# Sparse attention, MLP and routed experts on one core: denominators behind the first strikes, early outputs copied a step later, the next expert split two tiles ahead, ScalarE preparing the first tile's mask in every step

## The chip, the core and the metric

One core of one Trainium2 chip. The metric is the device time of one launch in microseconds; the median of several runs counts. TensorE multiplies matrices, VectorE (DVE in the rows), ScalarE (ACT) and GpSimd (POOL) work element by element, SyncE (SP) issues transfers. "Granted clock" is TensorE's clock as a share of its full 2.4 GHz; its other level is 1.2 GHz.

## What is computed

```python
# attention: q, k, v are 4 x 8 x 576 x 64
scores = scale * np.matmul(q, k.transpose(0, 1, 3, 2))
kth = np.partition(scores, -32, axis=-1)[..., -32:-31]
mask = scores >= kth
attn = exp(where(mask, scores, -1e9) - max);  attn /= attn.sum(-1)
x = (attn @ v), rows of 8 heads x 64 = 512, 2304 tokens
# MLP, 512 -> 2048 -> 512
h = x @ w_in;  g = maximum(h, 0) + log1p(exp(-abs(h)));  x = g @ w_out
# experts: 8, one per token by argmax of x @ w_gate, 512 -> 1024 -> 512
out[mask] = gate_w[mask] * (maximum(x[mask] @ w1[e], 0) @ w2[e])
```

Everything is float32. Large products are made of three: each operand is split into a rounded high part and the rest, its low part, and high x high, high x low and low x high are added.

## The kernel before

The scores are worked off in 72 blocks of 2 tiles (128 query rows x 576 keys each). A block passes the engines as a pipeline over steps i, written out by hand for each engine. In step i TensorE makes the scores of block i+1, transposes the probabilities of block i-2 (`turn_probs`, L536) and multiplies them with v (`times_v`, L554). ScalarE copies scores out (`scores_out`, L808), takes exponentials of block i-1 (`exponentials`, L823), multiplies block i-2 by its reciprocal denominators (`normalise`, L829), copies transposed probabilities (`probs_out`, `prT`, L836) and the output x (`x_out`, L843). VectorE finds the 32 largest scores of each row of block i: four rounds of the 8 largest (`maxima`, L1077), with those found struck out between rounds (`strike`, L1083). It also sums the exponentials and takes reciprocals (`reciprocals`, L1094 and L1097) and makes the low part of x (`x_low`, L1089). Its instructions run in the order in which they are written; so do those of every engine.

The mask that puts all but the 32 largest far below is made in one of two ways. GpSimd alone: compare and multiply (L1422, into `pr`), then add the scores (L1425). Or ScalarE first makes a large value for what lies below the limit (`cut_off`, L816) and GpSimd subtracts it (L1418). `cuts(n)` says which tiles of block n have the second way: both for n below 8, then tile 0 of even blocks, none of odd blocks. `tiles_of(n)` puts tile 1 first where only tile 0 is cut.

From step MLP_AT = 10 on the MLP runs in the same steps: group g of 256 tokens takes eight steps u = 0 to 7, one unit of the hidden layer each (`up`, `down`, on TensorE; `h_hi` on ScalarE L868, softplus and `h_lo` on GpSimd L1430 and L1436). `up(g, 0)` waits for the low part of the last block of its tokens (semaphore `x_split`). Steps 1 and 2 of the next group transpose two finished token tiles and compute their gate logits (`TURNS`); at step 0 of the next group ScalarE copies the group's result (`x2tok`, L889). Before step 10 ScalarE and GpSimd split the MLP's weights (L874, L880).

After the blocks come the routed experts. Tokens are sorted into tiles of 128 of one expert each; tile T has `rank_i[T]`, the place of its expert in the order. Tiles are gathered, multiplied (`e_up`, `e_down`, L669 to L671, with transposes of the hidden layer between, L699) and scattered by GpSimd (`scatter`: the indices are copied, L1517, then an indirect transfer is issued, L1520). Weights of the next expert are loaded into a second buffer; ScalarE casts their high part (`w_hi`, L912), VectorE makes the low part (`wbuf`, L1122). `next_expert(eng, T, split)` reads two ranks and does `split` if tile T+1 belongs to a later expert. In tile T ScalarE does `e_relu_out` (L947), `xs_out(T+1)`, the split of w1 and w2, `e_h_out` (`hrT_hi`, L953); VectorE does the low half of w1, `h_low` (L1271), the low half of w2, `relu(T+1)` (L1260), `xs_low(T+2)`, `y_out` (L1281). Here 19 tiles are in use, with two experts.

Of the kernel before, what the change touches and what calls it, by code (L numbers as in the profile page):

```python
# [20 lines left out]
def build(nc, q, k, v, w_in, w_out, w_gate, w1, w2, out):  # L21
# [68 lines left out]
    FREE = MLP_AT - 2  # L90

    def cuts(n):
        return (0, 1) if n < FREE else ((0,) if n % 2 == 0 else ())

    def cuts_before(n):
        return sum(len(cuts(x)) for x in range(n))
# [20 lines left out]
    with ExitStack() as ctx:  # L117
        def sb(name, shape, dt=F32):
            return ctx.enter_context(nc.sbuf_tensor(name, shape, dt))

        def sem(name):
            return ctx.enter_context(nc.semaphore(name))
# [121 lines left out]
        first_tile = sb("first_tile", [P, E])  # L244
        rank_e = sb("rank_e", [P, NTAB])
        rank_i = sb("rank_i", [P, COLS], I32)
        src_i = sb("src_i", [P, COLS], I32)
        dstf = sb("dstf", [P, NTAB])
        wrap = sb("wrap", [P, NTAB])
# [36 lines left out]
        lanes_ready, slots_raw, tables_ready = sem("lanes_ready"), sem("slots_raw"), sem("tables_ready")  # L286
        star_ready, tiles_ready, ranks_ready = sem("star_ready"), sem("tiles_ready"), sem("ranks_ready")
        onehot_ready = sem("onehot_ready")
        shift_ready = sem("shift_ready")
        xs_turned, xs_copied = sem("xs_turned"), sem("xs_copied")  # L290
        e_h_raw, e_relu, e_h_turned = sem("e_h_raw"), sem("e_relu"), sem("e_h_turned")
# [5 lines left out]
        def is_block(n):  # L297
            return 0 <= n < BLOCKS
# [34 lines left out]
        def next_expert(eng, T, split):  # L333

            rank, rank_next = (eng.value_load(rank_i[0:1, bass.ds(T + x, 1)], min_val=0,
                                              max_val=E - 1) for x in range(2))
            with eng.If(rank_next > rank):
                split(rank_next)

        def live_below(eng):  # L340
            tiles = eng.value_load(tend_i[0:1, E - 1:E], min_val=MOST, max_val=NTILE)
# [155 lines left out]
        def _(pe):  # L497
# [60 lines left out]

            def up(g, u, amid=()):
                n = UNITS * g + u  # L560
                if u == 0:
                    pe.wait_ge(x_split, PAIRS * 2 * (g + 1))
                if g == 0:
                    pe.wait_ge(wi_split, u + 1)
                if n:
                    pe.wait_ge(h_copied, n)
                if turns:
                    pe.wait_ge(logits_copied, turns)
                ps = psum[:, 5, 0:2 * WIDE].rearrange("p (a c) -> p a c", a=2)
                for part in range(2):  # L570
                    f = slice(part * P, (part + 1) * P)
                    for kk in range(KD):
                        if (part, kk) in amid:
                            amid[part, kk]()
                        first, last = kk == 0, kk == KD - 1
                        hi, lo = x_parts[:, g % 2, 0, kk, :], x_parts[:, g % 2, 1, kk, :]
                        nc.tensor.matmul(ps[:, part, :], wi_hi[:, u, kk, f], hi, start=first, stop=False)  # L577
                        nc.tensor.matmul(ps[:, part, :], wi_hi[:, u, kk, f], lo, start=False, stop=False)  # L578
                        mm = nc.tensor.matmul(ps[:, part, :], wi_lo[:, u, kk, f], hi,  # L579
                                              start=False, stop=last)  # L580
                mm.then_inc(h_raw, 1)
# [199 lines left out]
            turn_xs(1, 1)  # L781
            turn_h(0)
            e_up(1, rank_first)
            e_down(0, 0, rank_first, {KE // 2: slots_late, KE // 2 + 1: lambda: turn_h(1)}, halves=True)
            e_down(1, 1, rank_first, {KE - 2: lambda: turn_xs(2, 2)})
            pe.wait_ge(tiles_ready, 1)
            e_up(2)
# [15 lines left out]
        def _(act):  # L803
# [114 lines left out]
            def split_w2(rank):  # L918
                split_half(rank, w2_loaded, KD * EF, WLEN, w2_hi)

            def split(rank):
                split_w1(rank)
                split_w2(rank)

            def first_w1(n, half):
                at, rows = slice(n * 512, (n + 1) * 512), slice(half * KD // 2, (half + 1) * KD // 2)
                act.wait_ge(w1_loaded[0] if n else w1_first, 32)
# [31 lines left out]
            for i in range(-AHEAD, TAIL):  # L959
                now, late = is_block(i - 1), is_block(i - 2)  # L960
                if i < MLP_AT:
                    if late:
                        normalise(i - 2, 0)
                        normalise(i - 2, 1)
                    if now:
                        for t in cuts(i - 1):
                            cut_off(i - 1, t)
                    scores_out(i + AHEAD, 0)
                    scores_out(i + AHEAD, 1)
                    if late:  # L970
                        probs_out(i - 2, 0)
                    if wo_unit(i) is not None:
                        split_wo(wo_unit(i))
                    if now:
                        exponentials(i - 1, 0)
                    if late:
                        probs_out(i - 2, 1)
                    if now:
                        exponentials(i - 1, 1)
                    if wi_unit(i) is not None:  # L980
                        split_wi(wi_unit(i))
                    if late:
                        x_out(i - 2)
                    continue
                if up_at(i - 1):
                    h_high(*up_at(i - 1))
                if is_block(i + AHEAD):
                    scores_out(i + AHEAD, 0)
                    scores_out(i + AHEAD, 1)
                if late:  # L990
                    normalise(i - 2, 0)
                    normalise(i - 2, 1)
                if now:
                    for t in cuts(i - 1):
                        cut_off(i - 1, t)
                if up_at(i):
                    rectify(*up_at(i))
                if late:
                    probs_out(i - 2, 0)
                if now:  # L1000
                    exponentials(i - 1, 0)
                if late:
                    probs_out(i - 2, 1)
                if i in TURNS:
                    turn_out(TURNS[i][1], 5)
                if up_at(i):
                    logarithm(*up_at(i))
                if now:
                    exponentials(i - 1, 1)
                if down_at(i) and down_at(i)[1] == UNITS - 1:  # L1010
                    down_out(down_at(i)[0])
                if late:
                    x_out(i - 2)
                if i in TURNS:
                    logits_out(TURNS[i][1], 5)
# [37 lines left out]
            e_relu_out(1)  # L1053
            e_h_out(1)
            xs_out(2)
            act.wait_ge(tiles_ready, 1)
            next_expert(act, 1, split)
            _, live = live_below(act)

            def tile(T, place, live):  # L1060
                e_relu_out(T)
                with live(T + 1):
                    xs_out(T + 1)
                    next_expert(act, T, split)
                e_h_out(T)

            later_tiles(act, tile, live)

        @block.vector
        def _(dve):  # L1070
# [32 lines left out]
            for n in range(BLOCKS + 3):  # L1103
                for r in range(ROUNDS if is_block(n) else 1):
                    for t in range(2):
                        if is_block(n) and r:
                            strike(n, t, r)
                    if r == (1 if is_block(n) else 0) and is_block(n - 3):
                        x_low(n - 3)
                    for t in range(2):  # L1110
                        if is_block(n):
                            maxima(n, t, r)
                    if r == 0 and n > MLP_AT and is_block(n - 2):
                        reciprocals(n - 2)
                if 0 < n < MLP_AT:
                    reciprocals(n - 1)

# [258 lines left out]
            xs_low(2)  # L1376
            y_out(1, 1)

            dve.wait_ge(tiles_ready, 1)
            next_expert(dve, 1, split_w1)  # L1380
            next_expert(dve, 1, split_w2)
            relu(2)
            xs_low(3)
            _, live = live_below(dve)

            def tile(T, place, live):
                with live(T + 1):
                    next_expert(dve, T, split_w1)
                h_low(T)
                with live(T + 1):  # L1390
                    next_expert(dve, T, split_w2)
                    relu(T + 1)
                with live(T + 2):
                    xs_low(T + 2)
                y_out(T, place)
# [5 lines left out]
        def _(pool):  # L1401
# [108 lines left out]
                ).then_inc(gathered[par], 16)  # L1510

            def scatter(T, par):
                pool.wait_ge(e_y_copied, T + 1)
                if not (isinstance(T, int) and T == 0):
                    pool.wait_ge(scattered, T * 16)
                fixed(pool)
                nc.gpsimd.tensor_copy(dst_now[:], dst_i[:, bass.ds(T, 1)]).then_inc(dst_step, 1)  # L1517
                pool.wait_ge(dst_step, T + 1 + CREDIT)
                fixed(pool)
                nc.gpsimd.indirect_dma_start(  # L1520
                    out[:, :], bass.IndirectOffsetOnAxis(ap=dst_now[:], axis=0),
                    ys[:, par, :], None, bounds_check=TOK - 1, oob_is_err=False
                ).then_inc(scattered, 16)
# [53 lines left out]
```

## Time and profile before

| | us |
|---|---|
| median of 3 runs | 1127.15 (1124.67 to 1128.83) |
| profiled execution | 1126.63 |
| its span, first to last instruction | 1124.9 |
| PE busy | 1014.3 (90%) |
| DVE busy | 840.9 (75%) |
| ACT busy | 720.6 (64%) |
| POOL busy | 714.9 (64%) |
| mean granted TensorE clock | 0.961 |

The terms below are worked out from the profiled execution. "Idle before" in a row is how long the engine stood, and behind the arrow what it waited for. Shares over the whole span mix three stages: the first ten steps to about 120 us, the loop with the MLP to about 790 us, and the end of the MLP with the experts.

### The profile page before, as it was taken

Reading aid. Unit: us, or ns where it says so; the run is one execution under the profiler, and the core shown is the slowest. Engines: PE = TensorE matmul, PEld = TensorE weight load, DVE = VectorE, ACT = ScalarE, POOL = GpSimd, SP = SyncE. Lnnn points to the kernel's source line nnn. Section 1 sums busy time; section 2 is a strip of 40 time slices with the busy share of each in tenths; the row PEclk is TensorE's granted clock in tenths of the full one; section 3 lists DMA queues with packets and bytes.
Section 4 is the critical chain, followed back from the end, with each engine's and each line's share of the span. In section 5 each row is a group of like instructions: output and inputs, shape, how many; then the busy total and the mean of one; then the engine's idle time right before and its main releaser. Section 6 shows DMA issues by size and latency. Waiting matters only on the chain.

```text
span 1124.9 us, 21419 instructions
## 1 busy us (share of the span) xinstructions
PE 1014.3 (90%) x6951; PEld 815.3 (72%) x6952; DVE 840.9 (75%) x1850; ACT 720.6 (64%) x1339; POOL 714.9 (64%) x624
## 2 busy tenths in 40 slices
PE   3566899999999999899999999898998899999976
PEld 1343778787787787787778787787887788888864
DVE  6989999999999999999989999996244522222241
ACT  3777778888888888888878887887554111111230
POOL 3678788788788788788778888888351211112100
PEclk9756899999999999999999999999999999999988
DMA  9523125433324443323344332332481421111100
GB/s 326 212 89 144 68 101 172 135 118 111 129 78 176 133 138 113 113 94 113 136 156 139 111 113 94 114 114 105 140 308 66 160 84 49 37 37 47 37 9 19
DMA packets 42109, 130.46 MB, mean 116 GB/s; under 512 B 4064, under 2 KB 17376, under 8 KB 31776
## 3 DMA queue, kind: packets, MB, share of 16 engines
q1 hardware_dynamic: 38976, 119.57, 30.2%
q0 software_dynamic: 3040, 9.70, 2.6%
q8 instruction: 52, 0.85, 0.3%
q14 instruction: 41, 0.34, 0.1%
HBM read 111.43 MB, written 18.09 MB: 115 GB/s over the span
## 4 chain that ended last, share of the span: by engine, by line
PE 46%; POOL 29%; ACT 9%; issue 9%; DVE 4%; DMA 1%; SPq 1%; DVEq 0%; ACTq 0%; POOLq 0%
POOL pr L1422 12%; PE psum L669 7%; PE psum L671 6%; PE psum L670 6%; POOL pr L1425 6%; POOL h_lo L1436 4%; PE psum L554 4%; POOL hs L1430 4%; PE psum L536 3%; PE psum L520 3%; PE psum L577 2%; PE psum L596 2%; ACT h_hi L868 2%; POOL pr L1418 2%; PE psum L597 2%
## 5 line engine op out<-in xcount | busy, mean ns | idle before, releaser
L1077 DVE MAX8 top<-work 128x8 f32<-128x576 f32 x432 | 304.8, 747 | 0.0
L1422 POOL TENSOR_SCALAR pr<-sc,top 128x576 f32<-128x576 f32 x96 | 213.6, 2225 | 9.6
L1083 DVE MATCH_REPLACE8 work<-top,work 128x576 f32<-128x576 f32 x288 | 211.8, 743 | 0.0
L577 PE MATMUL psum<-x_parts,wi_hi 128*128 128x256 f32 x576 | 170.9, 297 | 11.9 <-DVE x_parts L1089 11.9
L578 PE MATMUL psum<-x_parts,wi_hi 128*128 128x256 f32 x576 | 163.6, 284 | 0.0
L579 PE MATMUL psum<-x_parts,wi_lo 128*128 128x256 f32 x576 | 163.4, 284 | 0.0
L536 PE MATMUL psum<-ident,pr 128*128 128x128 f32 (+1 forms) x720 | 112.2, 290 | 48.1 <-ACT prT L836 21.0
L823 ACT ACTIVATE pr<-pr,bias 128x576 f32<-128x576 f32 x144 | 111.6, 775 | 54.5 <-POOL pr L1425 53.4
L1425 POOL TENSOR_TENSOR pr<-pr,sc 128x576 f32<-128x576 f32 x96 | 136.5, 1422 | 8.0
L1430 POOL TENSOR_TENSOR hs<-hs,ab 128x512 f32<-128x512 f32 x72 | 92.8, 1290 | 76.5 <-ACT ab L860 76.4
L577 PEld LDWEIGHTS psum<-x_parts,wi_hi 128*128 128x128 f32 x576 | 110.8, 192 | 37.6 <-issue 21.3
L536 PEld LDWEIGHTS psum<-ident,pr 128*128 128x128 f32 (+1 forms) x720 | 78.7, 141 | 81.1 <-issue 76.2
L554 PE MATMUL psum<-prT,vtok 128*64 128x128 f32 (+3 forms) x1600 | 117.1, 287 | 12.6 <-ACT prT L836 12.6
L596 PE MATMUL psum<-wo_ring,h_hi 128*128 x288 | 125.0, 434 | 3.3 <-POOL h_lo L1436 3.1
L554 PEld LDWEIGHTS psum<-prT,vtok 128*64 128x64 f32 (+1 forms) x1600 | 85.7, 144 | 53.6 <-issue 32.1
L520 PE MATMUL psum<-kT,qT 64*128 64x288 f32 (+1 forms) x640 | 109.1, 464 | 9.8 <-ACT sc L808 9.0
L1436 POOL TENSOR_TENSOR h_lo<-hs,h_hi 128x512 fp32r<-128x512 f32 x72 | 93.1, 1293 | 34.2 <-ACT h_hi L868 32.5
L598 PE MATMUL psum<-wo_ring,h_lo 128*128 x288 | 114.5, 397 | 0.0
L597 PE MATMUL psum<-wo_ring,h_hi 128*128 x288 | 113.9, 395 | 0.0
L578 PEld LDWEIGHTS psum<-x_parts,wi_hi 128*128 128x128 f32 x576 | 111.1, 193 | 0.2
L579 PEld LDWEIGHTS psum<-x_parts,wi_lo 128*128 128x128 f32 x576 | 111.0, 193 | 0.0
L1517 POOL COPY dst_now<-dst_i 128x1 int32 (+1 forms) x19 | 3.5, 183 | 167.0 <-DVE ys L1281 167.0
(193 smaller groups left out, 2160.9 us busy)
## 6 DMA issues: line engine op xcount, KB each, us to landing
wo_ring<-wo_parts SPq DMA_DIRECT2D x72, 1024.0 KB, 4.8
wo_parts<-wo_ring SPq DMA_DIRECT2D x8, 1024.0 KB, 3.8
kT<-in_k SPq DMA_DIRECT2D x16, 288.0 KB, 3.3
qT<-in_q SPq DMA_DIRECT2D x16, 288.0 KB, 4.2
vtok<-in_v SPq DMA_DIRECT2D x16, 256.0 KB, 3.0
wo_raw<-in_moe_w_out SPq DMA_DIRECT2D x1, 4096.0 KB, 14.6
wi_raw<-in_moe_w_in SPq DMA_DIRECT2D x4, 1024.0 KB, 14.0
x_rows<-x2tok SPq DMA_DIRECT2D x16, 256.0 KB, 2.6
```

What stands on the lines that cost most here:

```text
L520: mm = nc.tensor.matmul(psum[rows, 2 * part + t, 0:HALF], qT[h * HD:(h + 1) * HD, p, cols], kT[h * HD:(h + 1) * HD, p, keys], start=True, ...
L536: mm = nc.tensor.transpose(transit[0:keys, c, :], pr[:, n % 2 * 2 + t, c * P:c * P + keys], ident[:])
L554: mm = nc.tensor.matmul(psum[h * HD:(h + 1) * HD, 4, cols], vtok[0:keys, p, c, h * HD:(h + 1) * HD], probs, start=(c == 0), stop=(c == FULL))
L577: nc.tensor.matmul(ps[:, part, :], wi_hi[:, u, kk, f], hi, start=first, stop=False)
L578: nc.tensor.matmul(ps[:, part, :], wi_hi[:, u, kk, f], lo, start=False, stop=False)
L579: mm = nc.tensor.matmul(ps[:, part, :], wi_lo[:, u, kk, f], hi, start=False, stop=last)
L596: nc.tensor.matmul(psum[:, 6 + a, :], high, hi, start=(f == 0), stop=False)
L1077: nc.vector.max(top[:, at, 8 * r:8 * r + 8], sc[:, at, :] if r == 0 else work[:, t, :]).then_inc(topk_step, 1)
L1083: nc.vector.match_replace(work[:, t, :], top[:, at, 8 * r - 8:8 * r], sc[:, at, :] if r == 1 else work[:, t, :], TAKEN).then_inc(topk_step, 1)
L1422: nc.gpsimd.tensor_scalar(to, sc[:, at, :], top[:, at, TOPK - 1:TOPK], OUT, ALU.is_lt, ALU.mult).then_inc(mask_step, 1)
L1425: nc.gpsimd.tensor_tensor(to, to, sc[:, at, :], ALU.add).then_inc(masked, 1)
L1436: nc.gpsimd.tensor_tensor(h_lo[:, n % 2], hs[:, n % 2], h_hi[:, n % 2].bitcast(F32), ALU.subtract).then_inc(h_ready, 1)
```

## The change

It does six things. (1) `cuts`: tile 0 of odd blocks too is cut by ScalarE. (2) VectorE's `reciprocals(n - 2)` stand behind the two first strikes of block n, ahead of `x_low`, from block 11 on. (3) In steps before 10 ScalarE's `x_out` of a block stands a step later, behind the normalisation. (4) `up(g, 0)` waits for all but one low part of x, and for the last only at the rows of x_parts that hold it. (5) w1 of the next expert is split in the tile two ahead of its first, found from a table `split_i` that VectorE makes with ten small instructions; w2 one ahead, as before; both behind `e_h_out` and `h_low`. The matmuls for the slots (L648) stand one product earlier in tile 0. (6) `scatter` copies its indices before it waits for y.

```diff
     def cuts(n):
-        return (0, 1) if n < FREE else ((0,) if n % 2 == 0 else ())
+        return (0, 1) if n < FREE else (0,)
...
+        def early_split(eng, T, split):
+            rank = eng.value_load(split_i[0:1, bass.ds(T, 1)], min_val=0, max_val=E - 1)
+            with eng.If(rank > 0):
+                split(rank)
...
             def up(g, u, amid=()):
                 n = UNITS * g + u
+
+                steps_x = PAIRS * 2 * (g + 1)
+                k_last = KD - 1 if PIECES[2 * g + 1][0] == "full" else KD // 2
                 if u == 0:
-                    pe.wait_ge(x_split, PAIRS * 2 * (g + 1))
+                    pe.wait_ge(x_split, steps_x - 1)
...
+                        if u == 0 and (part, kk) == (0, k_last):
+                            pe.wait_ge(x_split, steps_x)
...
-            e_down(0, 0, rank_first, {KE // 2: slots_late, KE // 2 + 1: lambda: turn_h(1)}, halves=True)
+            e_down(0, 0, rank_first, {KE // 2 - 1: slots_late, KE // 2: lambda: turn_h(1)}, halves=True)
...
                         normalise(i - 2, 0)
                         normalise(i - 2, 1)
+                    if is_block(i - 3):
+                        x_out(i - 3)
...
-                    if late:
+                    if i == MLP_AT - 1:
                         x_out(i - 2)
                     continue
...
                 e_relu_out(T)
                 with live(T + 1):
                     xs_out(T + 1)
-                    next_expert(act, T, split)
                 e_h_out(T)
+                early_split(act, T, split_w1)
+                with live(T + 1):
+                    next_expert(act, T, split_w2)
...
-                    if r == (1 if is_block(n) else 0) and is_block(n - 3):
-                        x_low(n - 3)
+                    if r == (1 if is_block(n) else 0):
+                        if n > MLP_AT and is_block(n - 2):
+                            reciprocals(n - 2)
+                        if is_block(n - 3):
+                            x_low(n - 3)
                     for t in range(2):
                         if is_block(n):
                             maxima(n, t, r)
-                    if r == 0 and n > MLP_AT and is_block(n - 2):
-                        reciprocals(n - 2)
...
             def tile(T, place, live):
-                with live(T + 1):
-                    next_expert(dve, T, split_w1)
                 h_low(T)
+                early_split(dve, T, split_w1)
                 with live(T + 1):
                     next_expert(dve, T, split_w2)
                     relu(T + 1)
...
             def scatter(T, par):
-                pool.wait_ge(e_y_copied, T + 1)
                 if not (isinstance(T, int) and T == 0):
                     pool.wait_ge(scattered, T * 16)
                 fixed(pool)
                 nc.gpsimd.tensor_copy(dst_now[:], dst_i[:, bass.ds(T, 1)]).then_inc(dst_step, 1)
                 pool.wait_ge(dst_step, T + 1 + CREDIT)
+                pool.wait_ge(e_y_copied, T + 1)
```

VectorE, start of block 12, before (`top` are the maxima, `work` the scores with strikes, `den` and `rden` the denominators and their reciprocals, `x_parts` the low part of x):

```order
L1077 MAX top<-sc 128x8 x2
L1094 TENSOR_REDUCE den<-eps 128x2
L1097 RECIPROCAL rden<-den 128x2
L1083 MATCH_REPLACE work<-top,sc 128x576 x2
L1089 TENSOR_TENSOR x_parts<-psum,x_parts 128x128
```

and after:

```order
L1095 MAX top<-sc 128x8 x2
L1101 MATCH_REPLACE work<-top,sc 128x576 x2
L1112 TENSOR_REDUCE den<-eps 128x2
L1115 RECIPROCAL rden<-den 128x2
L1107 TENSOR_TENSOR x_parts<-psum,x_parts 128x128
```

The two strikes now stand ahead of the sum of the exponentials.

ScalarE, a step of the loop that masks an odd block, before:

```order
L868 CAST h_hi<-hs 128x512
L808 ACTIVATE sc<-psum 128x576 x2
L829 ACTIVATE pr<-pr,rden 128x576 x2
L851 ACTIVATE ab<-psum 128x512
L852 ACTIVATE hs<-psum 128x512
L836 COPY prT<-psum 128x5x128
L823 ACTIVATE pr,eps<-pr,bias 128x576
```

and after:

```order
L885 CAST h_hi<-hs 128x512
L825 ACTIVATE sc<-psum 128x576 x2
L846 ACTIVATE pr<-pr,rden 128x576 x2
L833 ACTIVATE pr<-sc,bias 128x576
L868 ACTIVATE ab<-psum 128x512
L869 ACTIVATE hs<-psum 128x512
L853 COPY prT<-psum 128x5x128
L840 ACTIVATE pr,eps<-pr,bias 128x576
```

One activation, the cut, is new between the normalisation and the copies of the hidden unit.

ScalarE, the end of a tile in the experts' loop, before (`rank_i` is the table of ranks, `w_hi<-wbuf` a split, `hrT_hi` the transposed hidden layer):

```order
L335 TENSOR_LOAD rank_i
L335 ISA x3
L335 TENSOR_LOAD rank_i
L335 ISA x2
L337 COMPARE_AND_BRANCH
L909 ISA
L910 ISA
L912 ISA
L912 COPY w_hi<-wbuf 128x4096
L912 ISA
L912 COPY w_hi<-wbuf 128x4096
L337 UNCONDITIONAL_BRANCH
```

and after:

```order
L966 CAST hrT_hi<-psum 128x1024
L348 ISA
L348 TENSOR_LOAD split_i
L348 ISA x2
L349 COMPARE_AND_BRANCH
L926 ISA
L927 ISA
L929 ISA
L929 COPY w_hi<-wbuf 128x4096
L349 UNCONDITIONAL_BRANCH
L356 COMPARE_AND_BRANCH
L342 REGISTER_ALU
```

Before, both splits hang on one comparison of ranks and stand ahead of `hrT_hi`; after, the split of w1 hangs on `split_i` and stands behind `hrT_hi`, and that of w2 follows with a comparison of its own.

## Rows read from the trace of the kernel before

**Rows 1.** The page: the span.

```profile
span 1124.9 us, 21419 instructions
```

**Rows 2.** Three groups: length, busy PE, PEld, DVE, ACT, POOL; clock, DMA share, GB/s.

```profile
298.07:382.97 84.90, 80.55 (x618) 64.82 (x617) 80.98 (x185) 71.04 (x139) 72.37 (x56) 1.00 0.38 135
467.91:554.03 86.12, 81.80 (x620) 66.12 (x618) 80.97 (x185) 70.83 (x138) 72.38 (x57) 0.98 0.30 105
554.03:641.31 87.28, 85.12 (x729) 68.67 (x727) 81.07 (x185) 71.63 (x139) 72.42 (x56) 1.00 0.42 144
```

**Rows 3.** Waits, 128 to 790 us: total, times, longest.

```profile
ACT pr L823 <- POOL pr L1425: 53.4, 68, 2.2
...
DVE den L1094 <- ACT pr L823: 31.2, 38, 1.8
```

**Rows 4.** Busy time in four single steps, same columns.

```profile
455.56:467.19 11.63, 9.91 (x77) 7.83 (x75) 10.98 (x27) 9.21 (x19) 10.48 (x9) 1.00 0.15 64
477.66:488.71 11.05, 11.05 (x88) 9.17 (x90) 9.94 (x24) 9.08 (x20) 10.04 (x8) 1.00 0.26 98
509.69:519.62 9.93, 9.06 (x70) 7.00 (x68) 9.93 (x23) 8.77 (x18) 8.09 (x8) 1.00 0.22 69
519.62:530.54 10.92, 10.71 (x83) 8.67 (x82) 10.29 (x26) 8.34 (x16) 9.98 (x7) 1.00 0.39 149
```

**Rows 5.** Timeline of two steps, by engine: start, length, instruction, [idle before].

```profile
509.41 0.16 DVE L1094 TENSOR_REDUCE den<-eps 128x2 f32<-128x4 f32 x1 [0.80 <-ACT pr L823]
...
512.62 0.77 ACT L816 ACTIVATE pr<-sc,bias 128x576 f32<-128x576 f32 x1
...
515.60 0.78 ACT L823 ACTIVATE pr<-pr,bias 128x576 f32<-128x576 f32 x1 [0.65 <-POOL pr L1425]
...
518.20 1.40 DVE L1077 MAX8 top<-sc 128x8 f32<-128x576 f32 x2
...
521.22 1.44 ACT L829 ACTIVATE pr<-pr,rden 128x576 f32<-128x576 f32 x2
...
525.56 2.22 POOL L1422 TENSOR_SCALAR pr<-sc,top 128x576 f32<-128x576 f32 x1
```

**Rows 6.** Timeline: start of a group, TensorE; end of step 1, ScalarE.

```profile
457.49 0.39 PE L577 MATMUL psum<-x_parts,wi_hi 128*128 128x256 f32 x1 [1.72 <-DVE x_parts L1089]
...
477.60 0.17 ACT L900 COPY lg<-psum 128x8 f32<-128x8 f32 x1 [0.43 <-PE psum L617]
```

**Rows 7.** Timeline of an early step, ScalarE and TensorE.

```profile
59.44 1.04 ACT L880 CAST wi_hi<-wi_raw 128x1024 fp32r<-128x1024 f32 x1
...
61.44 2.29 PE L520 MATMUL psum<-kT,qT 64*128 64x288 f32 x8
...
61.56 0.27 ACT L843 CAST x_parts<-psum 128x128 fp32r<-128x128 f32 x1 [1.08 <-PE psum L554]
...
64.39 1.17 ACT L808 ACTIVATE sc<-psum 128x576 f32<-128x576 f32 x2
```

**Rows 8.** Busy time in two tiles of the routed stage.

```profile
1059.45:1071.86 12.41, 12.41 (x61) 10.25 (x60) 3.36 (x4) 5.66 (x5) 1.20 (x2) 1.00 0.05 21
1071.86:1093.60 21.74, 15.42 (x61) 12.33 (x60) 12.03 (x6) 5.55 (x5) 1.19 (x2) 0.84 0.03 12
```

**Rows 9.** Timeline, routed stage: tile 2, the switch of expert, the last scatter.

```profile
896.81 0.69 DVE L1260 TENSOR_SCALAR hr<-psum 128x512 f32<-128x512 f32 x1 [5.22 <-PE psum L671]
...
1060.60 1.02 ACT L953 CAST hrT_hi<-psum 128x1024 fp32r<-128x1024 f32 x1 [5.92 <-PE psum L699]
...
1068.29 7.13 ACT L912 CAST w_hi<-wbuf  x2 [1.20 <-issue]
...
1074.40 4.43 DVE L1122 TENSOR_TENSOR wbuf<-wbuf,w_hi  x1 [1.48 <-issue]
...
1079.22 0.79 PE L669 MATMUL psum<-w_hi,xsT_hi 128*128 x1 [6.32 <-DVE wbuf L1122]
...
1118.82 0.99 POOL L1520 DMA_INDIRECT out<-ys,dst_now  x1 [0.88 <-POOL dst_now L1517]
```

More of the change, by code:

```diff
@@ L246, in build @@
         rank_i = sb("rank_i", [P, COLS], I32)
+        last_rank = sb("last_rank", [P, 1])
+        rank_up = sb("rank_up", [P, NTAB])
+        step_up = sb("step_up", [P, NTAB - 1])
+        soon = sb("soon", [P, NTAB - 3])
+        alone = sb("alone", [P, NTAB - 3])
+        split_i = sb("split_i", [P, COLS], I32)
         src_i = sb("src_i", [P, COLS], I32)
@@ L288, in build @@
         onehot_ready = sem("onehot_ready")
+        splits_ready = sem("splits_ready")
         shift_ready = sem("shift_ready")
@@ L919, in split_w2 @@
                 split_half(rank, w2_loaded, KD * EF, WLEN, w2_hi)
-            def split(rank):
-                split_w1(rank)
-                split_w2(rank)
             def first_w1(n, half):
@@ L1055, in _ @@
             xs_out(2)
-            act.wait_ge(tiles_ready, 1)
-            next_expert(act, 1, split)
+            act.wait_ge(splits_ready, 1)
+            early_split(act, 1, split_w1)
+            next_expert(act, 1, split_w2)
             _, live = live_below(act)
@@ L1377, in _ @@
             y_out(1, 1)
-            dve.wait_ge(tiles_ready, 1)
-            next_expert(dve, 1, split_w1)
+            then(nc.vector.tensor_scalar(last_rank[:], rank_of[:, E - 1:E], -1.0, None, ALU.add))
+            then(nc.vector.tensor_scalar(rank_up[:], rank_e[:], last_rank[:, 0:1], None, ALU.min))
+            then(nc.vector.tensor_tensor(step_up[:], rank_up[:, 1:NTAB], rank_up[:, 0:NTAB - 1],
+                                         ALU.subtract))
+            then(nc.vector.tensor_scalar(step_up[:, 0:1], step_up[:, 0:1], 0.0, 1.0, ALU.mult, ALU.add))
+            at0, at1, at2 = (slice(x, NTAB - 3 + x) for x in range(3))
+            then(nc.vector.tensor_scalar(soon[:], step_up[:, at1], -1.0, 1.0, ALU.mult, ALU.add))
+            then(nc.vector.tensor_tensor(soon[:], soon[:], step_up[:, at2], ALU.mult))
+            then(nc.vector.tensor_tensor(soon[:], soon[:], rank_up[:, 3:NTAB], ALU.mult))
+            then(nc.vector.tensor_tensor(alone[:], step_up[:, at0], step_up[:, at1], ALU.mult))
+            then(nc.vector.tensor_tensor(alone[:], alone[:], rank_up[:, 2:NTAB - 1], ALU.mult))
+            nc.vector.tensor_tensor(split_i[:, 1:NTAB - 2], soon[:], alone[:], ALU.add
+                                    ).then_inc(splits_ready, 1)
+            dve.wait_ge(splits_ready, 1)
+            early_split(dve, 1, split_w1)
             next_expert(dve, 1, split_w2)
```

## Prediction

> **What bounds the kernel now.** I read the page first: a span of 1124.9 us [rows 1] in which no engine is saturated throughout. So the stages were read apart. The softmax/MLP loop (steps 10 to 73, about 120 to 790 us) is the largest. Cut at the starts of its eight-step groups, an undisturbed group takes 84.90 us, in which VectorE is busy 80.98, ScalarE 71.04, GpSimd 72.37 [rows 2]: 10.61 us a step against 10.12 of VectorE work. The chain of waits over the loop names two things: ScalarE's exponentials wait 53.4 us in 68 places for GpSimd's mask, and VectorE's denominators wait 31.2 us in 38 places for those exponentials [rows 3]. Nearly all of VectorE's gaps are that second wait.
>
> I cut the steps where ScalarE starts `h_hi`. There are two kinds, in turn. From 509.69 to 519.62 (9.93 us) ScalarE prepares tile 0's mask itself; from 519.62 to 530.54 (10.92 us) it doesn't, and GpSimd is busy 9.98 us, its gaps only those between instructions [rows 4]: a second compare (2.22 us, at 525.56) stands ahead of softplus, the biases and the next low half [rows 5]. In the short one the cycle runs `h_hi`, low half, one compare and addition, exponential (it waits 0.65 for them), `prT` copy, exp and ln, softplus, `h_hi`, each as the one ahead ends. That cycle over ScalarE and GpSimd, 9.93 us, is left as it is.
>
> **The change, part by part.**
>
> *Masks.* Every odd block loses one 2.22 us compare on GpSimd and gains a 0.77 us activation on ScalarE (at 512.62) [rows 5]. A long step becomes a copy of the short one, which already holds the 0.77: 10.92 - 9.93 = 0.99 us less [rows 4], if nothing else comes last. In the short step the cut ends before the `prT` copy and the exponential behind it still waits 0.65 for GpSimd, so that wait is the cover; without it the cut would cost up to 0.77.
>
> *Denominators.* They pass the two first strikes. One stood waiting at 509.41 for 0.80 us; the strikes are about 1.4 us of work, more than that wait, so the gaps, 0.8 us in the mean [rows 3], should close [rows 5]. The reciprocal lands later: in the block at 518.20, start + 1.4 (maxima) + 1.4 (strikes) + 0.3 = 521.3, while ScalarE's normalisation starts at 521.22 [rows 5]. That is 0.1 late, inside the 0.65 of slack. VectorE can run nearly 2 us further ahead before it meets the exponentials again, and does, since its work is 10.12 a step against more than that in the steps below. Queued behind the waiting denominators are the low half `x_low` and all later maxima; they get earlier.
>
> Not every long step gains. In a group the steps are u = 0 to 7. Steps 1 and 2 also transpose and gate a token tile on TensorE. There ScalarE's last instruction, the logits copy, waits for TensorE (477.60, 0.43 us) and `h_hi` starts right behind it [rows 6]; step 2 (477.66 to 488.71) is a long one, but TensorE is busy all its 11.05 us [rows 4], so it gains nothing and loses about 0.1 to the cut. Step 0 gains: TensorE waited 1.72 us for `x_low` at 457.49 [rows 6]; now the first 9 of its 12 matmuls of the first part pass ahead and `x_low` is earlier, and ScalarE's 9.21 us, which hold the `x2tok` copies, with the cut's 0.77 and the 0.65 of waiting make 10.6 against 11.63 [rows 4]. So a normal group wins at steps 0, 4 and 6: 3 x 0.99 - 0.1 = 2.9 us, giving 82.0, still above VectorE's 81.0. I count three such steps in five groups, two in each of the first (no group behind it), the sixth (more TensorE work: its row has 85.12 us busy in 87.28) and the last: 21 steps, 20.8 us, less 0.7 = 20.1. The fifth group is 86.12 long against 84.90 with a granted clock of 0.98 [rows 2]: TensorE fell to 1.2 GHz for a while behind its wait for `x_low`. I take that 1.2 back too. **Loop: 21 us.** Bounds: 0, where the cut eats the gain, and 31.2, where all denominators' waits go.
>
> *Early outputs.* In steps 2 to 8 ScalarE's wi cast ends at 60.48, then it stands 1.08 us until P.V ends to copy x, then normalises, cuts twice and copies scores. Moved a step later, the normalisation starts at 60.5 and the copy and cuts end at 63.6; but the scores that come next are written only at 63.73 [rows 7], so the score copy moves from 64.39 to about 63.75: 0.6 us. Six such steps: 3.6 us. `x_low` reads the copy behind the first strikes, 2.8 us into its block; the copy is ready before that. With 0.5, a guess, for the first loop step: **4 us**; bounds 0 and the whole 1.08 in each of seven steps, 7.6.
>
> *Expert split.* The routed stage runs 12.41 us a tile on TensorE without a gap, except once: the tile in which the second expert begins takes 21.74, at a clock of 0.84 [rows 8]. ScalarE casts w1 and w2 in one piece of 7.13 us, VectorE makes w1's low half only behind the previous tile's output (4.43 us), TensorE waits 6.32 us and comes back slow (0.79 us for its first matmul) [rows 9]. 21.74 - 12.41 = 9.33 us is what the whole disturbance costs; the 3.0 beyond the wait are mostly the clock's and go with it, since the stalls left are short. Now w1 is split a tile earlier and w2 where it was. What is late next is VectorE's `relu`, queued behind each low half: ScalarE has `hrT_hi` ready at 1061.62, casts w1 from about 0.8 later (one table load; two took 1.20) for 3.57, VectorE's low half ends near 1070.5, two loads 1.48 and `relu` 0.69 give 1072.7, and TensorE wants it at 1071.86 [rows 8, 9]: 0.8 late; a tile later, with w2, 0.6 by the same sum. **9.3 - 1.4 = 7.9 us**, bounds 6 and 9.3. The ten small instructions that make the table (about 0.2 us each) and the wait for it stand in VectorE's 5.22 us of idle ahead of tile 2's `relu` at 896.81 [rows 9]; without that cover they would cost 2 us. Moving the slot matmuls one product ahead costs at most 0.1: they only just find their input ready, and what follows waits for tile 0's product anyway.
>
> *Last scatter.* The index copy passes the wait for y. The issue stands 0.88 us behind that copy at the end [rows 9]; I take 0.5 off the last scatter, bounds 0 and 1.3.
>
> **Sum.** 21 + 4 + 7.9 + 0.5 = 33.4 us off the profiled execution's 1126.63 us (its span and 1.7 around it): 1093.2. The median is 0.5 above that execution, so I say **1093 us**.
>
> **Rivals.**
> (a) *VectorE dense.* Every denominators' wait goes and the ScalarE/GpSimd cycle gives way; the loop is worth 31.2 and the sum is 1083. For it: 80.98 of 84.90 busy. Against: the 9.93 cycle and TensorE's full steps stand in the timeline. The Trainium skill, Perfetto Trace Analysis, Identifying the Most-Contended Engine, would have the engine with the highest occupancy and the gaps on it decide, and this is the outcome it gives. By the trace a cycle over two less busy engines decides instead.
> (b) *The cut isn't hidden.* With a cut in every step ScalarE's queue has no light step left in which to catch up, each cut holds rectify and `prT` copies, and TensorE's second transposes wait (a cut step has 9.06 us of TensorE work in 9.93 now, and the room shrinks). 21 steps then win 0.3 instead of 0.99: loop 6 to 7 us, about 1108.
> (c) *Late denominators, slower.* If VectorE stays the last (10.12 against 9.93 a step), its blocks start nearer to `h_hi` than 1.4 us, and each normalisation, with all of ScalarE's work behind it, starts late. It decides once the block starts within about 0.8 us of `h_hi`. At 0.2 us the normalisation is 1.3 late, 0.65 of it hidden, 0.65 x 63 = 41 lost against 33 gained with the loop's 21: 1135. Against: steps 0 to 2 of each group take over 31 us, VectorE 30.4, so it regains what five lighter steps cost it.
> (d) *Little.* Something else ends both kinds of step, and only the tail's 8 and some of the start's 4 stay: 1116; with (c) at a fraction it could come to nothing.
>
> **Numbers.** Forecast (1086 to 1101 by its bounds) 0.60; (a) 0.13; (b) 0.14; (d) 0.07; (c) 0.06. Leaving out the far ends of (a), (c) and (d) gives 1083 to 1109. About 0.5% is what a measurement tells from no change. Faster by more: 0.90, within it 0.04, slower 0.06.
>
> **What the profile would show.** A normal group at 82 us with no long steps; exponentials waiting for masks under 1 us everywhere; denominators waiting only in the steps that gate; the ScalarE copy of x behind the normalisation with no wait; no 1.2 GHz stretch at the expert switch, and two gaps under 1 us before `turn_h`. Denominators' reciprocals followed at once by a waiting normalisation in most steps would prove (c); `prT` copies that end behind the masks would prove (b).

## The result, and the profile after

The changed kernel takes 1089.51 us (median of 4 runs, 1088.79 to 1090.97) against 1126.45 for the kernel before on the same chip: a ratio of 0.9672 (0.965 to 0.9695). The forecast was 1093. Its profiled execution took 1088.8 us, 37.8 less than that of before. The page's head answers to [rows 1]:

```profile
span 1087.1 us, 21522 instructions
...
PE 1008.0 (93%) x6951; PEld 811.8 (75%) x6952; DVE 841.1 (77%) x1860; ACT 736.4 (68%) x1371; POOL 651.5 (60%) x624
```

ScalarE gained 16 us of work, GpSimd lost 63. I cut the execution at three places that both traces hold (GpSimd's first `h_lo` in the loop, the last block's, the first behind them): 4.0 us came before the loop, 24.9 in it, 0.7 in the last units of the MLP, 8.2 in the routed stage. The loop's share is firm: in the four traces with exactly this loop it takes 636.5 to 637.1 us. Ahead of it and in the routed stage, executions of the same code lie up to 3 us apart. The windows of after, two groups and then four steps (columns as in [rows 2]), answer to [rows 2, 4]:

```profile
276.93:358.62 81.69, 80.15 (x618) 64.88 (x616) 81.11 (x185) 72.86 (x142) 64.48 (x56) 1.00 0.38 132
522.01:606.12 84.11, 83.86 (x724) 68.04 (x724) 81.00 (x185) 73.14 (x143) 64.44 (x56) 1.00 0.43 147
440.32:450.65 10.33, 10.13 (x78) 8.06 (x77) 10.29 (x25) 9.63 (x20) 8.31 (x9) 1.00 0.18 74
461.11:472.16 11.05, 11.05 (x88) 9.16 (x90) 10.79 (x25) 9.63 (x20) 8.42 (x9) 1.00 0.30 110
492.15:502.10 9.95, 9.88 (x78) 7.76 (x74) 9.95 (x23) 8.77 (x17) 8.07 (x7) 1.00 0.32 114
502.10:512.06 9.96, 9.69 (x76) 7.74 (x74) 9.93 (x23) 8.77 (x17) 8.06 (x7) 1.00 0.29 105
```

The long steps are gone: 10.92 became 9.96. Step 0 fell from 11.63 to 10.33, step 2 stayed at 11.05, where TensorE is busy throughout. VectorE has 0.6 us left in a group where it had 3.9. In the last two rows it is busy throughout: a plain step (4 to 7) takes less time than the 10.1 us of work that VectorE has in a step, so it falls behind there and catches up in steps 0 to 2. So busy time alone doesn't say what ends a plain step; the last experiment does. The waits between 124 and 761 us, where [rows 3] showed 53.4 and 31.2:

```profile
POOL hs L1464 <- ACT ab L877: 100.1, 62, 2.9
...
ACT pr L840 <- POOL pr L1459: 27.9, 44, 1.8
...
DVE den L1112 <- ACT pr L840: 17.0, 14, 9.4
```

Of VectorE's 17.0, 9.4 is one wait behind the last block. GpSimd now waits for ScalarE, ScalarE for GpSimd, each in turn: the cycle. The timeline of one block (columns as in [rows 5]):

```profile
499.21 1.40 DVE L1095 MAX8 top<-sc 128x8 f32<-128x576 f32 x2
...
501.98 0.14 DVE L1112 TENSOR_REDUCE den<-eps 128x2 f32<-128x4 f32 x1
502.15 0.17 DVE L1115 RECIPROCAL rden<-den 128x2 f32<-128x2 f32 x1
```

```profile
503.71 1.44 ACT L846 ACTIVATE pr<-pr,rden 128x576 f32<-128x576 f32 x2
505.04 0.77 ACT L833 ACTIVATE pr<-sc,bias 128x576 f32<-128x576 f32 x1
...
506.66 0.71 ACT L853 COPY prT<-psum 128x640 f32<-128x640 f32 x1
...
508.03 0.78 ACT L840 ACTIVATE pr<-pr,bias 128x576 f32<-128x576 f32 x1 [0.66 <-POOL pr L1459]
```

The first group of rows is VectorE's, the second ScalarE's. The block starts 2.9 us ahead of `h_hi` (502.11); the reciprocals are ready 1.4 us before the normalisation, which waits for nothing, and the exponential still waits 0.66 for the mask, as in [rows 5]. In the early steps x is copied without a wait, and the score copy of [rows 7] no longer waits for ScalarE's own queue but 0.44 us for TensorE's scores, as forecast:

```profile
60.20 0.25 ACT L860 CAST x_parts<-psum 128x128 fp32r<-128x128 f32 x1
60.34 1.45 ACT L833 ACTIVATE pr<-sc,bias 128x576 f32<-128x576 f32 x2
62.23 1.19 ACT L825 ACTIVATE sc<-psum 128x576 f32<-128x576 f32 x2 [0.44 <-PE psum L532]
```

The routed stage, windows of the two tiles in which the second expert's w1 and w2 are split [rows 8], and timeline rows of that stretch and of the last scatter [rows 9]:

```profile
1030.13:1042.55 12.42, 12.42 (x62) 10.25 (x61) 7.60 (x5) 5.72 (x4) 1.20 (x2) 1.00 0.05 21
1042.55:1055.50 12.95, 12.58 (x61) 10.11 (x59) 7.06 (x5) 5.61 (x4) 1.19 (x2) 1.00 0.05 20
```

```profile
1032.51 3.63 ACT L929 CAST w_hi<-wbuf  x1 [0.22 <-issue]
...
1046.39 3.63 ACT L929 CAST w_hi<-wbuf  x1 [1.69 <-issue]
...
1036.50 4.42 DVE L1141 TENSOR_TENSOR wbuf<-wbuf,w_hi  x1 [2.95 <-ACT w_hi L929]
1040.84 0.68 DVE L1279 TENSOR_SCALAR hr<-psum 128x512 f32<-128x512 f32 x1
...
1055.50 1.10 PE L716 MATMUL psum<-ident,hr 128*128 128x128 f32 x8 [0.38 <-DVE hr L1279]
...
1080.99 0.98 POOL L1554 DMA_INDIRECT out<-ys,dst_now  x1 [7.79 <-DVE ys L1300]
```

Where 21.74 us stood now stand 12.95, at full clock. `relu` at 1040.84 starts directly behind the low half and ends 1.0 us before the tile does. In the tile of 12.95, w2's, `relu` comes too late: TensorE waits 0.38 us for it.

### The profile page after: what moved, and what is told of

Same layout as the page of the kernel before. It is cut to its first block, busy times and chain, and to the rows that moved or that the text cites. A ratio compares the mean times of both kernels' runs of the same rounds, so it can differ in the third digit from the quotient of the medians.

```text
span 1087.1 us, 21522 instructions
## 1 busy us (share of the span) xinstructions
PE 1008.0 (93%) x6951; PEld 811.8 (75%) x6952; DVE 841.1 (77%) x1860; ACT 736.4 (68%) x1371; POOL 651.5 (60%) x624
## 4 chain that ended last, share of the span: by engine, by line
PE 52%; POOL 25%; ACT 10%; issue 9%; DMA 1%; SPq 1%; DVE 1%; ACTq 0%; POOLq 0%; DVEq 0%
POOL pr L1456 7%; PE psum L686 6%; PE psum L688 6%; PE psum L687 6%; PE psum L566 6%; POOL pr L1459 5%; POOL h_lo L1470 5%; PE psum L532 4%; POOL hs L1464 4%; POOL pr L1452 4%; PE psum L548 3%; PE psum L594 3%; PE psum L613 3%; PE psum L615 2%; PE psum L614 2%
## 5 line engine op out<-in xcount | busy, mean ns | idle before, releaser
L1456 POOL TENSOR_SCALAR pr<-sc,top 128x576 f32<-128x576 f32 x64 | 142.5, 2227 | 6.4
L548 PE MATMUL psum<-ident,pr 128*128 128x128 f32 (+1 forms) x720 | 109.8, 286 | 36.2 <-ACT prT L853 16.1
L566 PEld LDWEIGHTS psum<-prT,vtok 128*64 128x64 f32 (+1 forms) x1600 | 85.7, 144 | 51.5 <-issue 31.2
L1452 POOL TENSOR_TENSOR pr<-sc,pr 128x576 f32<-128x576 f32 x80 | 113.7, 1426 | 16.9 <-ACT pr L833 16.9
L1554 POOL DMA_INDIRECT out<-ys,dst_now x19 | 19.2, 1012 | 162.9 <-DVE ys L1300 162.9
L853 ACT COPY prT<-psum 128x640 f32<-128x640 f32 x144 | 99.7, 692 | 12.0 <-PE psum L548 12.0
```

Of the source, the lines that this page charges most:

```text
L548: mm = nc.tensor.transpose(transit[0:keys, c, :], pr[:, n % 2 * 2 + t, c * P:c * P + keys], ident[:])
L566: mm = nc.tensor.matmul(psum[h * HD:(h + 1) * HD, 4, cols], vtok[0:keys, p, c, h * HD:(h + 1) * HD], probs, start=(c == 0), stop=(c == FULL))
L1452: nc.gpsimd.tensor_tensor(to, sc[:, at, :], to, ALU.subtract).then_inc(masked, 1)
L1456: nc.gpsimd.tensor_scalar(to, sc[:, at, :], top[:, at, TOPK - 1:TOPK], OUT, ALU.is_lt, ALU.mult).then_inc(mask_step, 1)
```

## The experiments

Each ratio below is against the kernel before, timed on the same chip; differences to the changed kernel go by its 1089.5. The kernel before had medians of 1126.2, 1125.3 and 1127.3 us beside the three sets of experiments, so a difference under 2 us tells nothing. The changed kernel itself, run again beside the last set, gave 1089.52:

> The changed kernel itself, beside the three others on the same chip: 1089 to 1090.

**Masks as before.** In the changed kernel `cuts` is what it was.

```diff
-        return (0, 1) if n < FREE else (0,)
+        return (0, 1) if n < FREE else ((0,) if n % 2 == 0 else ())
```

> The changed kernel with the masks as before: tile 0 of odd blocks made by GpSimd alone, all else changed. My account: the second compare makes odd steps 10.9 us again, so nearly all of the loop's 25 us is lost and a normal group goes from 81.7 back to about 84.5; sum 1089.5 + 20 to 24 = 1110 to 1113. Rival (the denominators' waits were what bound, VectorE dense): the denominators no longer wait, so the group stays near 82 and the time under 1095.

1110.62 us, 0.9864 (0.9841 to 0.9887): 21.1 lost. A group is 84.90 again, step 0 (the second row) 11.61, with everything else of the change in place:

```profile
378.69:463.59 84.90, 80.85 (x618) 64.99 (x617) 80.96 (x184) 71.00 (x140) 72.29 (x56) 1.00 0.35 117
451.98:463.59 11.61, 11.41 (x89) 9.38 (x88) 10.35 (x25) 9.19 (x19) 10.43 (x9) 1.00 0.15 63
```

```profile
461.71 0.78 ACT L840 ACTIVATE pr<-pr,bias 128x576 f32<-128x576 f32 x1 [1.17 <-POOL pr L1459]
```

In that step GpSimd makes two compares and is busy 10.43 us. ScalarE's second exponential waits 1.17 us for the mask behind them, and the `x2tok` copies and `h_hi` stand behind it in ScalarE's queue. VectorE's waits are back too, although its reciprocals stand behind the strikes: 25.6 us in 32 places, without the one wait of 10.7 behind the last block. The cut carries the loop.

**Reciprocals as before**, and **the whole wait for x_low back at `up(g, 0)`**, each in the changed kernel.

```diff
-                        if n > MLP_AT and is_block(n - 2):
-                            reciprocals(n - 2)
...
+                    if r == 0 and n > MLP_AT and is_block(n - 2):
+                        reciprocals(n - 2)
```

> The changed kernel with the reciprocals ahead of the first strikes as before. My account: the cycle over ScalarE and GpSimd (9.95 us a step) binds, not VectorE, and with the short masks VectorE can still start its block 1.9 us ahead of h_hi instead of 3.3, so little is lost where VectorE's 10.12 of work must be caught up: 0 to 6 us, 1090 to 1096. Rival (denominators bind): VectorE's waits of about 0.8 us come back in some 38 places, 1115 to 1120.

```diff
-                    pe.wait_ge(x_split, steps_x - 1)
+                    pe.wait_ge(x_split, steps_x)
```

> The changed kernel with the first up product of a group waiting for all low parts of x, as before. The kernel with the masks alone kept 11.4 us in step 0 where the changed one has 10.3. My account now: this wait, not the denominators, makes the difference; step 0 goes from 10.3 to about 11.2 and the time to 1096 to 1100. Rival (in the full change VectorE runs far enough ahead that x_low is done in time): under 1 us, 1090.

1088.98 (0.9672, 0.965 to 0.9695) and 1088.70 (0.966, 0.9642 to 0.9678): neither costs anything that can be told. Undisturbed groups are 81.8 long in both. With the reciprocals first, VectorE waits 11.6 us in 19 places; with the whole wait, TensorE waits up to 0.9 at a group's start. Both hide.

**One part alone, in the kernel before:** the masks, and the reciprocals.

```diff
-        return (0, 1) if n < FREE else ((0,) if n % 2 == 0 else ())
+        return (0, 1) if n < FREE else (0,)
```

> The kernel before with one edit: ScalarE cuts tile 0 of every block from step 10 on. My account: this edit carries the loop; a normal group goes from 84.9 to within 0.5 us of 81.7, and the time falls by 22 to 25 us, to 1101 to 1104. Rival (the masks need the denominators behind the strikes, or the split wait of the up product, to pay): the group stays at 83.5 or above and the gain is under 12 us.

> The kernel before with one edit: the reciprocals behind the first strikes. My account: GpSimd's odd steps stay 10.9 us, VectorE's waits only move to another place; a normal group stays at 84.9 and the time falls by 0 to 2 us, 1124 to 1126. Rival (VectorE's waits bind): the group falls by 2 us or more, 1105 to 1112.

Masks alone: 1112.54, 0.9877 (0.9848 to 0.9906), some 14 us, less than undoing them costs. Reciprocals alone: 1123.86, 0.9978 (0.9964 to 0.9992), some 2.5 us, 1 to 4 by the interval. An undisturbed group is still 84.95. The profiled executions lie 1.9 apart: 1.1 by the loop's first `h_hi`, and 0.8 behind it, where the fifth group's dip in the clock (86.12 to 84.96) and 0.5 in the sixth were won and 0.7 lost in the first. The denominators still wait, 26.0 us in 32 places without the one behind the last block, where they waited 31.2 in 38: passing the strikes hardly shortens their waits. The plain steps of masks alone are 9.95, but step 0 is 11.43, a group 82.8, and once 84.25 at a clock of 0.98. TensorE's waits there and the start of the product in the step 0 that ends the 84.25 group say why:

```profile
PE psum L577 <- DVE x_parts L1089: 10.5, 7, 1.9
```

```profile
366.97 0.39 PE L577 MATMUL psum<-x_parts,wi_hi 128*128 128x256 f32 x1 [1.89 <-DVE x_parts L1089]
...
368.26 0.28 PE L578 MATMUL psum<-x_parts,wi_hi 128*128 128x256 f32 x1
368.38 0.36 PE L579 MATMUL psum<-x_parts,wi_lo 128*128 128x256 f32 x1
368.54 0.42 PE L577 MATMUL psum<-x_parts,wi_hi 128*128 128x256 f32 x1
```

It waits 1.89 us, and 1.4 us later the clock falls: matmuls of 0.28 us last 0.42.

**Masks and the later wait alone.** As the one before, with `up`'s wait split.

```diff
-                    pe.wait_ge(x_split, PAIRS * 2 * (g + 1))
+                    pe.wait_ge(x_split, steps_x - 1)
...
+                        if u == 0 and (part, kk) == (0, k_last):
+                            pe.wait_ge(x_split, steps_x)
```

> The kernel before with two edits: the masks, and the up product that waits for the last low part of x only at its rows. My account: these two are the whole of the loop's gain; a normal group at 81.7 to 81.9 us, 1100 to 1103. Rival (the denominators are needed too): groups at 82.3 or above, 1105 or more.

1101.21, 0.9774 (0.9757 to 0.9791): 11.3 faster than masks alone (11.6 by the ratios; the two ran on different chips). Undisturbed groups 81.72 to 81.78, step 0 10.33, TensorE's waits for x_low 2.5 us in 5 places, at most 0.6. These are the changed kernel's groups, with the reciprocals where they stood. The split wait and the later reciprocals stand in for each other: masks need one of them, and the second is worth nothing that can be told.

**x copied in its own step before step 10**, in the changed kernel.

```diff
-                    if is_block(i - 3):
-                        x_out(i - 3)
...
-                    if i == MLP_AT - 1:
+                    if late:
                         x_out(i - 2)
```

> The changed kernel with x copied in the same step before step 10, as before. My account: the 0.4 to 1.1 us waits per early step come back, 5.2 us by step 9, of which the changed kernel later lost 1.2 to a slow clock in the first up product: 3.5 to 5 us more, 1093 to 1095. Rival (early steps hidden behind the weights' loading and splitting): no more than 1 us, 1090.

1093.36, 0.9703 (0.9679 to 0.9727): 3.9 lost. The copy waits 1.09 again. The profiled executions lie 6.0 apart, all of it by the loop's first `h_hi` (129.42 against 123.42). That is one pair. Over all kept traces `h_hi` starts at 123.6 us in the mean of the nine kernels that copy x a step later (122.3 to 125.6), and at 127.4 in the five that don't (125.9 to 129.4): 3.8 apart, as the medians say.

**One split of both weights**, in the changed kernel.

```diff
                 with live(T + 1):
                     xs_out(T + 1)
+                    next_expert(act, T, split)
                 e_h_out(T)
-                early_split(act, T, split_w1)
-                with live(T + 1):
-                    next_expert(act, T, split_w2)
...
+                with live(T + 1):
+                    next_expert(dve, T, split_w1)
                 h_low(T)
-                early_split(dve, T, split_w1)
```

> The changed kernel with the split of w1 in the tile before its first use and ahead of hrT_hi, as before (the table is still made). Both accounts: the tile of the switch is 21.7 us again, 8.8 us more, 1098. If the clock's part does not come back with the wait it is 6.3 us more, 1096.

1096.91, 0.9732 (0.9707 to 0.9757): 7.4 lost. TensorE waits the 6.32 of [rows 9] again:

```profile
1051.50 0.79 PE L686 MATMUL psum<-w_hi,xsT_hi 128*128 x1 [6.32 <-DVE wbuf L1141]
```

**How much cover the cut has.** A second cut of 0.77 us (0.67 net of overlap) ahead of the real one, into unused memory, in 61 blocks of the changed kernel.

```diff
+                if n > MLP_AT:
+                    if n > MLP_AT + 1:
+                        act.wait_ge(again, n - MLP_AT - 1)
+                    nc.scalar.activation(gap_b[:, 0:SEQ], sc[:, n % 3 * 2 + t, :], ACT.Relu,
+                                         bias=bias[:, n % 2, 1, t:t + 1], scale=-FAR).then_inc(again, 1)
```

> The changed kernel with a second, useless cut of the same shape on ScalarE in each of 61 blocks (0.67 us of queue time each; its result is read by nobody). My account: ScalarE waits for the mask by 0.65 us in a plain step and a quarter of it in others, so most is hidden: 0 to 0.2 us a plain step, 0.7 in the steps in which ScalarE runs dense (step 0), together 5 to 15 us: 1095 to 1105. Rival (the cut is not hidden): 61 x 0.67 = 41 us, 1130.

1118.59, 0.9929 (0.9902 to 0.9956): 29.1 lost, far above what I expected. A plain step went from 9.95 to 10.28, steps 1 to 3 grew by the full 0.67. The exponential's wait for GpSimd fell to 0.7 us in all, and TensorE's transposes wait instead, 37.3 us where the changed kernel has 7.8:

```profile
PE psum L549 <- ACT prT L859: 37.3, 61, 1.3
```

So the cover was some 0.3 to 0.4 us in a plain step, half of the 0.65 that the wait shows, and none in steps 1 to 3. By these waits TensorE stands where ScalarE's copies come late. Rival (b)'s mechanism exists, one cut further on.

**Reciprocals behind the second strikes**, in the changed kernel.

```diff
-                    if r == (1 if is_block(n) else 0):
-                        if n > MLP_AT and is_block(n - 2):
-                            reciprocals(n - 2)
-                        if is_block(n - 3):
-                            x_low(n - 3)
+                    if r == (1 if is_block(n) else 0) and is_block(n - 3):
+                        x_low(n - 3)
+                    if r == (2 if is_block(n) else 0) and n > MLP_AT and is_block(n - 2):
+                        reciprocals(n - 2)
```

> The changed kernel with the reciprocals behind the second strikes, 2.8 us of VectorE work later than now. It asks what late denominators cost: VectorE starts its block up to 3.3 us ahead of h_hi, so reciprocals come about 2.6 us behind h_hi and the normalisation, due at 1.6, is 1.0 late; 0.65 is hidden. My account: 0.3 to 0.8 us a step, 15 to 40 us in all, 1105 to 1130, with ScalarE waiting for rden. Rival (TensorE and ScalarE have more slack than that): under 5 us, 1094.

1150.44, 1.0205 (1.017 to 1.024): 61 us more than the changed kernel, and slower than the one before. ScalarE's and then VectorE's waits, 120 to 770 us:

```profile
ACT pr L846 <- DVE rden L1115: 60.2, 55, 1.8
...
DVE x_parts L1107 <- ACT x_parts L860: 63.0, 58, 1.8
```

VectorE now waits for x, whose copy stands behind the normalisation that waits for VectorE. By these waits that loop holds a plain step, now 11.0 to 11.04 us.

**GpSimd's remaining compare ahead of the low half**, in the changed kernel: tile 1's compare needs only the maxima, so it may stand before `h_lo`.

```diff
+                ahead = up_at(i - 1) and is_block(i - 1)
+                if ahead:
+                    compare(i - 1, 1)
                 if up_at(i - 1):
...
-                        mask(i - 1, t)
+                        mask(i - 1, t, ahead and t == 1)
```

> A new version: the changed kernel with GpSimd's compare for tile 1 ahead of the low half of the hidden unit instead of behind it, so that it runs while ScalarE still makes h_hi. My account: the cycle over ScalarE and GpSimd loses about 0.5 us of its 9.95, and then VectorE's work binds (81.0 a group against 81.7): 2 to 5 us less, 1085 to 1088. Rival: the low half comes 1.7 us later and TensorE's down product waits for it, 0 to 5 us more, 1090 to 1095.

1084.82, 0.9628 (0.9611 to 0.9644): 4.7 faster than the changed kernel, and the fastest here. A plain step falls to 9.84, by 0.11 where I expected 0.5, and an undisturbed group to 81.2:

```profile
367.08:448.28 81.20, 80.75 (x620) 65.15 (x616) 80.74 (x185) 74.16 (x143) 64.17 (x57) 1.00 0.38 126
```

```profile
489.69 0.62 ACT L885 CAST h_hi<-hs 128x512 fp32r<-128x512 f32 x1 [0.22 <-POOL hs L1469]
...
490.37 2.23 POOL L1450 TENSOR_SCALAR pr<-sc,top 128x576 f32<-128x576 f32 x1
492.67 1.29 POOL L1475 TENSOR_TENSOR h_lo<-hs,h_hi 128x512 fp32r<-128x512 f32 x1
493.92 1.44 POOL L1464 TENSOR_TENSOR pr<-pr,sc 128x576 f32<-128x576 f32 x1
```

The compare did not leave the cycle. It starts as `h_hi` ends, so it runs in the low half's place and the low half behind it; what left the cycle is the pass over `h_hi`. From the start of softplus to that of the first exponential it takes 7.07 us instead of 7.23. No work of VectorE's changed, so the shorter step shows that this cycle, not VectorE, ended it. What ends the 9.84 was not tried. The whole gain is not explained by it: of the 4.0 us between the profiled executions of the two kernels on this chip, 1.7 lie in the loop's eight groups, 0.6 ahead of them and 1.7 behind them, where the edit does nothing.

## Why the prediction was right, step by step

- **Masks: right, and the term that decides.** The long step became the short one (10.92 to 9.96, forecast 9.93). The cycle over ScalarE and GpSimd ends a plain step: a second compare in it makes 10.92 of 9.96, in either kernel, and another order of GpSimd's instructions alone makes 9.84.
- **Loop, 21 us: mis-sized, 24.9 measured.** A normal group is 81.7, not 82.0, since step 0 won 1.3 instead of 1.0. The first group and the sixth, in each of which I had counted two winning steps, won 3.0 and 3.2: the 85.12 of TensorE work that I read as the sixth group's floor [rows 2] is not one, since the window now shows 83.86 of 84.11. The fifth won the same 3.2 and the clock's 1.2 (86.12 to 81.7), as forecast.
- **Denominators: the lateness was forecast right as harmless, the worth of the move wrongly attributed.** The reciprocals are 1.4 early. The gaps closed, but not because the denominators pass the strikes, as I had it: with the move and long steps they wait 26.0 us in 32 places (25.6 with all of the change but the masks), with short steps and no move 11.6 in 19, with both 7.6 in 13, each without the one wait of about 10 behind the last block. The move alone gave 2.5 us, and beside the masks and the split wait nothing. What I read as step 0's gain from the move is the split wait's just as well.
- **The cut's cover: right for what was asked of it, smaller than I read.** I took the 0.65 wait for it; the doubled cut shows 0.3 to 0.4.
- **Early outputs, 4: right.** 4.0 by the stages, 3.9 by undoing it. The sum is right partly by luck: the x copies were 5.2 earlier by step 9, and some 1.2 went again when TensorE's first up product ran at 1.2 GHz. Over all kept traces that product starts 4.7 us earlier with the early outputs and takes 0.9 longer (below).
- **Expert switch, 7.9: right within 1.** The tile gave 8.8, the w1 tile nothing (12.42), undoing the split cost 7.4. The tile of w2's split is 0.5 long, with `relu` late, instead of 0.8 and 0.6 in two tiles: the two loads that I priced at 1.48 between low half and `relu` take no time of their own, and w1's cast starts 0.22 behind `hrT_hi` instead of 0.8. The ten small instructions cost nothing visible.
- **Last scatter, 0.5: right, by the trace alone.** From the end of y's copy to the issue stand 0.87 us, before 1.38. It was not tried by itself, nor were the slot matmuls.
- **Rival (a)** gave 1083 for a loop worth 31.2. VectorE's waits weren't that worth, yet VectorE came close to dense: 81.1 of 81.7. The Trainium skill, Perfetto Trace Analysis, Identifying the Most-Contended Engine, would have sent a reader to the engine with the highest occupancy; in a group of the kernel before that was VectorE. By the runs, moving what it waited for gave 2.5 us alone and nothing on top of the rest, while taking 63 us of work from GpSimd, one of the two least busy of the four, gave 14 alone and 21 on top of the rest. **Rival (b)** didn't come; its wait appears with a second cut. **Rival (c)** didn't come: a block starts 2.9 us ahead of `h_hi`. One round later the mechanism costs 61 us, more than the 41 that I priced. I had not seen the loop over x_low that feeds it. **Rival (d)** didn't come.

Of the expectations, four missed: masks alone gave less, the whole wait cost less, the doubled cut and the later reciprocals cost more. Two more came near in time, but not as I had it: reciprocals alone gave a little more than 0 to 2, and the compare ahead took 0.11 off a plain step instead of 0.5. The terms that stand add up: masks with the split wait 1101.2, less 7.4 and 3.9, is 1089.9. Open is why the first product so often runs slow behind the early outputs, and what ends the 9.84.

## What to carry to other kernels

Cut a loop into its kinds of step before costing an edit, and look in each for the cycle of waits: here it ran over two engines that were busy 71 and 72 us of 85, and the waits of VectorE, busy 81, were its shadow. Two edits that each remove the same wait are worth one; it took runs with one part alone, in either kernel, to show that. A wait that seems to be an edit's cover can be worth less than its length, here half, when other engines are fed by what stands behind it, so double the edit and see.

## What the runs showed of the hardware

The same product can run at either level of the clock. Before, TensorE's first up product of the loop began at 117.93 us, and after 1.2 us its matmuls fell from 0.41 to 0.28 us each. After, it began at 112.67, and they stayed at 0.41 for 3.8 us:

```profile
112.67 0.58 PE L594 MATMUL psum<-x_parts,wi_hi 128*128 128x256 f32 x1
...
115.40 0.41 PE L594 MATMUL psum<-x_parts,wi_hi 128*128 128x256 f32 x1
```

The product took 4.9 us instead of 3.6. The earlier start doesn't settle it. With x copied in its own step the product began at 118.60, later than in the kernel before, and took 4.9 as well; in the changed kernel with one split of both weights it began at 115.15 and ran at 0.28 from its second matmul:

```profile
118.98 0.41 PE L595 MATMUL psum<-x_parts,wi_hi 128*128 128x256 f32 x1
```

```profile
115.37 0.28 PE L595 MATMUL psum<-x_parts,wi_hi 128*128 128x256 f32 x1
```

Of the nine profiled executions with the early outputs eight had the slow product (4.7 to 4.9 us), of the five without them one. TensorE had gaps in every step ahead of it in both kernels; which of them decides was not tried.

The other surprise is the register loads. Around two of them ScalarE stood 1.20 us before a cast and VectorE 1.48 [rows 9]; now the one behind `hrT_hi` left 0.22 idle, and those behind VectorE's low half left nothing: `relu` starts at 1040.84, where the low half of 4.42 us that began at 1036.50 ends. Between `hrT_hi` and w2's cast a tile later, with three loads and their branches behind a cast of 1.01 us, 1.69 are left. It looks as if loads run under the instruction ahead of them as far as it is long enough; no run tried this by itself.
